# Attention on one core: TensorE's order in a unit grouped by the shape of the weights, masks as four 64x64 products, turned weights signalled by bank

## The reference

```python
B, H, S, D = 4, 8, 576, 64            # factor = 4, scale = 1 / sqrt(D)
q_d, k_d, v_d = (mean over 4 tokens of q, k, v)
out_up = np.repeat(sm_attn(q_d, k_d, v_d), factor, axis=2)
mask = np.abs(pos[:, None] - pos[None, :]) < factor
scores = np.where(mask, scale * np.matmul(q, k.transpose(0, 1, 3, 2)), -1000000000.0)
out_local = np.matmul(softmax(scores), v)
x = (out_up + out_local) as (B * S, H * D)          # 2304 x 512
x = (sigmoid(x @ w_gate) * (x @ w_val)) @ w_out     # d_ff 1536
h = x @ w_in; out = (h * sigmoid(1.702 * h)) @ w_out2   # d_ff 2048
```

## Time and profile before

| what | value |
|---|---|
| median of 3 runs | 871.63 us (871.37 to 872.4) |
| profiled execution | 872.51 us, span 870.8 us |
| TensorE busy | 857.5 us (98%) |
| VectorE, ScalarE, GpSimd busy | 624.1, 487.0, 589.2 us |
| six transposes of `turn` and of `turn_out`, mean ns of one | 282, 281 |
| granted TensorE clock, mean | 0.998 |

### The profile page before, as it was taken

How to read it: one execution, slowest core, us unless ns; L and a number is a source line. 1 busy time by engine, 2 the same in 40 slices (tenths; PEclk the granted TensorE clock), 3 DMA queues, 4 the chain that set the end, 5 groups by cost and what they waited for, 6 DMA issues and landing times.

```text
span 870.8 us, 18384 instructions
## 1 busy us (share of the span) xinstructions
PE 857.5 (98%) x6638; PEld 832.2 (96%) x6638; DVE 624.1 (72%) x1140; ACT 487.0 (56%) x1083; POOL 589.2 (68%) x471
## 2 busy tenths in 40 slices
PE   8989999999999999999999999999999999999998
PEld 6878899999999999999999999999999999999998
DVE  5767645555658685967676877777888778878777
ACT  5778754545536364645354646654676466556652
POOL 6688788888758648785457776763668644846523
PEclk9999999999999999999999999999999999999999
DMA  9877466685955787838588825345246751636432
GB/s 329 264 211 218 166 242 237 223 342 204 382 172 192 294 287 292 301 109 285 210 274 305 285 91 205 97 147 195 67 174 218 266 183 59 218 123 230 171 120 73
DMA packets 77369, 184.26 MB, mean 212 GB/s; under 512 B 5856, under 2 KB 31456, under 8 KB 74464
## 3 DMA queue, kind: packets, MB, share of 16 engines
q1 hardware_dynamic: 77280, 183.10, 60.2%
HBM read 141.66 MB, written 41.42 MB: 210 GB/s over the span
## 4 chain that ended last, share of the span: by engine, by line
PE 94%; issue 2%; DVE 1%; ACT 1%; POOL 1%; DMA 1%; SPq 0%; ACTq 0%; DVEq 0%
PE o_ps L808 10%; PE o_ps L809 10%; PE o_ps L810 10%; PE d_ps L662 7%; PE d_ps L664 7%; PE d_ps L663 7%; PE s_ps L662 6%; PE o_ps L653 6%; PE s_ps L664 6%; PE s_ps L663 6%; PE t_ps L662 3%; PE t_ps L663 3%; PE t_ps L664 3%; PE o_ps L626 2%; PE t_ps L597 1%
## 5 line engine op out<-in xcount | busy, mean ns | idle before, releaser
L808 PE MATMUL o_ps<-g_hi,v 128*128 128x384 f32 x504 | 169.6, 337 | 0.6 <-DVE att L1773 0.5
L809 PE MATMUL o_ps<-g_lo,v 128*128 128x384 f32 x504 | 169.4, 336 | 0.0
L810 PE MATMUL o_ps<-g_hi,v 128*128 128x384 f32 x504 | 169.4, 336 | 0.0
L1773 DVE TENSOR_TENSOR att<-o_ps,att 128x384 f32<-128x384 f32 x212 | 118.1, 557 | 56.4 <-PE o_ps L810 53.8
L2123 POOL TENSOR_TENSOR v<-v_f,v 128x512 fp32r<-128x512 f32 x72 | 95.0, 1340 | 56.2 <-ACT v L1076 56.2
L2123 POOL TENSOR_TENSOR v<-raw,v 128x512 fp32r<-128x512 f32 x54 | 70.9, 1312 | 89.8 <-ACT v L1069 77.2
L662 PE MATMUL d_ps<-xs_hi,w 128*128 128x384 f32 x360 | 121.0, 336 | 2.0 <-issue 1.2
L664 PE MATMUL d_ps<-xs_hi,w 128*128 128x384 f32 x360 | 120.5, 335 | 0.0
L663 PE MATMUL d_ps<-xs_lo,w 128*128 128x384 f32 x360 | 120.4, 335 | 0.0
L662 PE MATMUL s_ps<-xs_hi,w 128*128 128x384 f32 x300 | 101.2, 337 | 1.3 <-POOL xs_lo L2153 1.3
L664 PE MATMUL s_ps<-xs_hi,w 128*128 128x384 f32 x300 | 100.5, 335 | 0.0
(11 more groups left out here) (186 smaller groups left out, 2099.6 us busy)
## 6 DMA issues: line engine op xcount, KB each, us to landing
w<-w_split SPq DMA_DIRECT2D x48, 768.0 KB, 7.0
w<-w_split SPq DMA_DIRECT2D x48, 512.0 KB, 7.8
w<-w_split SPq DMA_DIRECT2D x96, 256.0 KB, 5.3
w_split<-w SPq DMA_DIRECT2D x12, 1792.0 KB, 6.7
raw<-in_w_out_dram SPq DMA_DIRECT2D x36, 512.0 KB, 4.5
w_split<-job_w SPq DMA_DIRECT2D x8, 1792.0 KB, 7.7
vw<-in_v_win_dram SPq DMA_DIRECT2D x16, 390.0 KB, 4.6
raw<-in_w_gate_val_dram SPq DMA_DIRECT2D x24, 256.0 KB, 3.3
```

Source lines behind the costliest of these rows:

```text
L808: pe.matmul(bank, vh, gh, start=(start and k == c), stop=False, skip_group_check=True)
L809: pe.matmul(bank, vh, gl, start=False, stop=False, skip_group_check=True)
L810: mm = pe.matmul(bank, vl, gh, start=False, stop=(k == c + 1), skip_group_check=True)
L1773: vec.tensor_tensor(part, value, part, ALU.add).then_inc(y_added, 1)
```

## The change

`masks(u)` makes four products for a unit, for each head one to each half of the output partitions (weights 64x64), in place of two with 64x128. In the loop, `score(i + 2)` goes ahead of `turn(i + 1)`, so that TensorE's order is weigh, masks, score, turn, turn_out. `turn` fills bank 1 first (pairs 4 and 5) and then bank 0, and signals after each; `copy_turned` copies in the same order, waits for each bank by itself and signals each copy. The values of `turned` and `copied` are doubled in the waits, and `weigh_pooled`, which writes only bank 1, waits for the copy of bank 1 alone.

```diff
@@ -327,7 +327,7 @@
                     sp.wait_ge(halved, u - QK_SLOTS + 1)
                     sp.wait_ge(scored, u - QK_SLOTS + 1)
                 if u > QK_SLOTS:
-                    sp.wait_ge(turned, u - QK_SLOTS)
+                    sp.wait_ge(turned, 2 * (u - QK_SLOTS))
                 sp.dma_start(qk[slot][:, 0, PAD:PAD + S], q_t[u]).then_inc(qk_loaded[slot], 16)
 
             def load_k(u):
@@ -535,9 +535,11 @@
             def masks(u):
                 if u >= 1:
                     pe.wait_ge(shifted, u)
-                for h in range(2):
-                    rows = slice(h * HK, (h + 1) * HK)
-                    pe.matmul(s_ps[:, h, 0:PAIRS * KW], picks[rows, :], mask[rows, :, :], start=True, stop=False)
+                for par in range(2):
+                    out_rows = slice(par * HK, (par + 1) * HK)
+                    for h in range(2):
+                        rows = slice(h * HK, (h + 1) * HK)
+                        pe.matmul(s_ps[out_rows, h, 0:PAIRS * KW], picks[rows, out_rows], mask[rows, :, :], start=True, stop=False)
 
             def score(u):
 
@@ -593,13 +595,14 @@
                     pe.wait_ge(copied_d, u)
                 if u >= 2:
                     pe.wait_ge(od_ready, u - 1)
-                for pair in range(PAIRS):
+                for pair in (*range(PT0, PAIRS), *range(PT0)):
                     mm = pe.transpose(t_ps[:, pair // PT0, (pair % PT0) * P:(pair % PT0 + 1) * P], e[:, pair, :, :].rearrange("p h k -> p (h k)"), ident[:, :])
-                mm.then_inc(turned, 1)
+                    if pair in (PT0 - 1, PAIRS - 1):
+                        mm.then_inc(turned, 1)
 
             def turn_pooled(u):
                 pe.wait_ge(normed_d, u + 1)
-                pe.wait_ge(copied, u + 1)
+                pe.wait_ge(copied, 2 * u + 2)
                 if u == 0:
                     pe.wait_ge(v_summed, 2)
                 if u >= 1:
@@ -631,7 +634,7 @@
                 pe.wait_ge(copied_d, u + 1)
                 pe.wait_ge(v_summed, u + 1)
                 if u + 1 < UNITS:
-                    pe.wait_ge(copied, u + 2)
+                    pe.wait_ge(copied, 2 * u + 3)
                 for c in range(2):
                     for h in range(2):
                         rows = slice(h * D, (h + 1) * D)
@@ -876,8 +879,8 @@
             for i in range(1, UNITS - 2):
                 weigh(i)
                 masks(i + 2)
+                score(i + 2)
                 turn(i + 1)
-                score(i + 2)
                 turn_out(i)
                 weigh_pooled(i)
                 sum_values(i + 2)
@@ -975,15 +978,14 @@
                                ).then_inc(v_summed, 1)
 
             def copy_turned(u):
-                act.wait_ge(turned, u + 1)
                 if u == 0:
                     act.wait_ge(sums_turned, 1)
                 if u >= 1:
                     act.wait_ge(weighed, u)
-                for b, pairs in enumerate((range(PT0), range(PT0, PAIRS))):
-                    c = nc.scalar.copy(p_t[:, 2 * pairs.start:2 * pairs.stop, 0:QW],
-                                       t_ps[:, b, 0:len(pairs) * P].rearrange("p (w k) -> p w k", k=HK)[:, :, 0:QW])
-                c.then_inc(copied, 1)
+                for n, (b, pairs) in enumerate(((1, range(PT0, PAIRS)), (0, range(PT0)))):
+                    act.wait_ge(turned, 2 * u + n + 1)
+                    nc.scalar.copy(p_t[:, 2 * pairs.start:2 * pairs.stop, 0:QW],
+                                   t_ps[:, b, 0:len(pairs) * P].rearrange("p (w k) -> p w k", k=HK)[:, :, 0:QW]).then_inc(copied, 1)
 
             def copy_turned_pooled(u):
                 act.wait_ge(turned_d, u + 1)
@@ -1539,7 +1541,7 @@
                 scores = s_ps[:, :, 0:PAIRS * KW].rearrange("p h (a k) -> p h a k", k=KW)
                 dve.wait_ge(maxed, u + 1)
                 if u >= 1:
-                    dve.wait_ge(turned, u)
+                    dve.wait_ge(turned, 2 * u)
                 vec.tensor_tensor(e[:, :, :, 0:KW].rearrange("p a h k -> p h a k"), scores,
                                   nmax[:, :].rearrange("p (h a) -> p h a", h=2).unsqueeze(3).broadcast_to([P, 2, PAIRS, KW]),
                                   ALU.add).then_inc(shifted, 1)
```

## The result

The changed kernel takes 872.72 us (median of 22 runs, 871.49 to 875.62), beside 871.57 us for the kernel before in as many runs taken with them; the ratio is 1.0020, with an interval of 1.0012 to 1.0029. So it is about 0.2% slower, where 867.0 was forecast and 864.8 to 869.7 was the range. Its profiled execution took 872.78 us, with a span of 870.0 us.

What follows compares the result with a forecast made beforehand. The prediction took TensorE, busy 857.5 of 870.8 us, as the bound. 13 units x 0.37 = 4.8 us, plus 0.3 outside the loop, less 0.5 for GpSimd, took 4.6 from 871.63 to 867.0 us; range 864.8 to 869.7.

Steps and rivals of the forecast that it cites:

- The drains: TensorE's unit: three of four changes of weight shape saved, 0.10 to 0.15 us each, 0.30 to 0.45 us a unit.
- Masks as four products: Masks group: four products run side by side in four array quarters, at no added time.
- rival (c): Masks group: the four products do not run side by side, 5 us slower, 876.8 us; chance 0.07.
- rival (b): Masks' borders: fp32 to bf16 weights cost like a shape change, so only one is saved, 869.6 us; chance 0.09.
- The unit of 5.67: Attention loop: an undisturbed unit falls from 6.04 to 5.67 us, 0.37 us less.
- a floor of T+2.27: turn_out waits for VectorE's normalise, earliest 2.27 us after weigh's start (T); a unit gains 0.38 us at most.
- Rival (d): Loop: normalise's chain, or ScalarE in units with castings, holds a unit near 5.9 us, 869.5 us; chance 0.09.
- The loads of the masks: Mask weights of 64 columns lose the fast load, estimated 53 ns each; 0.7 us if exposed, expected to be hidden.
- The clock: TensorE's clock was read as granted in full in every slice.
- GpSimd: Two units' turn_pooled wait for GpSimd's late pooled multiplication, 0.10 and 0.38 us; 0.5 us lost in all.
- rival (a): The 2.3 us instruction-fetch stall vanishes, 865.1 us, chance 0.14; or another joins, 869.3 us, chance 0.06.
- the sum: Whole kernel: 4.8 us from the loop, plus 0.3 outside, less 0.5 for GpSimd: 4.6 us gained.

Runs made afterwards that it cites:

- changed kernel without streams: The changed kernel with q and k loaded for four units only and both forms of v for two: 867.38 us, ratio 0.9960.
- masks alone: The kernel before with the four 64x64 mask products and without the new order: 870.25 us, ratio 0.9993.
- order alone: The changed kernel with the masks as two products again, keeping the new order, split copies and signals: 875.73 us, ratio 1.0049.
- orders before and after without streams: The kernel before and the changed kernel, q and k loaded for four units only, v's forms for two: 867.89 and 867.38 us.
- long pause: The changed kernel without streams, with the masks in the loop waiting for the end of VectorE's normalisation: 886.21 us, ratio 1.0169.
- 64 added products: The changed kernel with 64 small products (128 instructions) put once behind the first score, ahead of the loop: 875.39 us, ratio 1.0050.
- added loads: The kernel before with v's windows of units 3 to 15 loaded a second time into unused space: 874.48 us, ratio 1.0034.
- without v's windows: The changed kernel with v's windows loaded for the first two units only: 873.93 us, ratio 1.0034.

## Why the prediction was wrong

**Right, and in size.** The drains: 0.09 to 0.11 us less for weigh, masks and turn, 0.04 and 0.03 for score and turn_out. Masks as four products: 0.14 us for the group, so they run side by side, and rival (c), the slower side of the forecast, was wrong. bf16 weights ahead of fp32 ones of one shape cost nothing (0.14 us from masks to score), so rival (b) was wrong as well. The Trainium skill, "TensorEngine Tiling (Array Packing)", section "Key Properties", says that the array drains at a change of tiling mode and not between tiles of one mode; the trace agrees, across the two types too, with 0.75 us from weigh to masks where it was 0.86. The unit of 5.67; turn_out at T+2.30, beside a floor of T+2.27 that no wait shows at work. Rival (d) was wrong.

**The loads of the masks.** One load of 64x64 in bf16 has 107 ns in the records, one of 64x128 had 93. The Trainium skill, "TensorE: Matmul & The Clock Gate", section "Weight-path perf modes", gives the fast load only to weights of a full 128 columns. By the same page's section "LDWEIGHTS (loading the stationary operand)", P/1.2, an estimate for 64 columns is 53 ns; neither recorded time is as short. What counts is the row of PEld in the undisturbed unit, where all four start at 60.28, beside weigh's last products, and none delays the masks:

```profile
60.28 0.13 PEld L542 LDWEIGHTS s_ps<-mask,picks 64*64 64x64 bf16 x4
```

**The clock.** The prediction read it as granted in full in every slice. The mean of that execution is 0.998, and 0.72 from 5 to 10 us; a slice is too coarse to show it. No term of the sum hangs on this.

**GpSimd, a term that did not come.** 0.5 us was counted for it. The changed kernel shows no wait for it, probably because each gap gives it the rest that it lacked; in the changed kernel without streams, which has no gap near that unit, turn_pooled waits for it once, 0.3 us.

**The step that failed** is rival (a), and with it the sum, in which the stalls for instructions stand at no change. Rival (a) named the cause rightly, a stall for instructions whose place depends on where TensorE stands, and then priced it as one throw of a die: the one stall goes, 2.3 us gained, or one joins, 2.3 us lost, with 0.06 for the second. Two things were not seen. First, I had one wait of the trace, and did not ask how near all the other borders were to stalling. At five more borders of the kernel before, from 36 to 98 us, TensorE came to the border 2.35 to 2.8 us after the fetch had begun, where it needs some 2.4: these pieces came just in time (one of them 0.23 us late). Second, the change itself takes away what these borders had to spare: it makes the order quicker to execute and by that quicker to run out of program, and its fetches start later as well. The added instructions, on which I put it, bring no gaps by themselves (masks alone: 1.9 us in the loop, before 2.8), while the order alone has 5.0; together they have 8.3. The loop lost 5.5 us there, where rival (a) had 2.3, and that is more than the 4.8 us that its units gained.

**What is open.** Why a fetch starts when it does. In the orders before and after without streams it starts from 0.3 us ahead of the border to 3.3 us behind it, mostly with 30 to 150 instructions of the piece done; with streams up to 5.9 us behind (in order alone). Why it starts later in the new order with no data on the queues is not known, and this is the larger part of the difference there. That transfers delay it is shown only by leaving all streams out (mean 2.10 to 1.15 us before, 2.53 to 1.78 after); leaving out 390 KB a unit, or adding as much, moved the mean of the kernel before by only 0.1 us (to 1.99 and 2.17). Which transfers, and where they meet, no run shows. Orders that save the changes of shape and still spread the small products were not tried. None of the kernels that compute everything was faster than before by more than its interval.

## What to carry to other kernels

- On a TensorE that is busy throughout, read its stream a second way, by instructions per us. A wait for "issue" that returns at a fixed count of instructions is the program arriving late. Here a piece of 256 needed about 2.4 us from the start of its fetch, and the fetch mostly started 1 to 4 us into the piece before. Without data, the orders in which some 256 pass in 4.2 us or less stalled, and the one with 4.4 did not.
- Grouping equal shapes saves about 0.1 us for each drain, but many small products in a row spend the program fastest. Before joining two such groups, count the instructions in both. Keeping a group of few, long products between them may help where the kernel already shows such a wait; no run here tried it beyond the order before itself.
- A single wait in a trace is the visible end of a distribution. Ask for all places of its kind how much they have to spare before pricing it as chance.

## What was not expected of the hardware

After some pauses and some gaps the clock fell. In the kernel with the long pause TensorE stood 1.35 us ahead of the masks at 51.27, and from then on the same groups took, from start to start, 1.09 for score, 1.34 for turn and 1.32 for turn_out, where they took 0.78, 0.71 and 0.75 in the unit at 44.01:

```profile
51.27 0.34 PE L546 MATMUL s_ps<-mask,picks 64*64 64x336 bf16 x4 [1.35 <-DVE o_tok L1561]
51.44 1.17 PE L557 MATMUL s_ps<-qk 64*48 64x56 f32 x48
52.53 1.54 PE L603 MATMUL t_ps<-ident,e 128*128 128x128 f32 x6
53.87 1.39 PE L653 MATMUL o_ps<-ident,o_tok 128*128 128x128 f32 x6
55.19 0.71 PE L645 MATMUL t_ps<-pd_t,v_sum 128*64 128x144 f32 x8
```

The window of it, with the granted clock as the last column but two:

```profile
51.30:54.90 3.60, 3.60 (x63) 3.47 (x64) 1.66 (x3) 1.23 (x6) 1.65 (x4) 0.54 0.70 219
```

0.54 is the lower level, 1.2 GHz, for nearly all of these 3.6 us, and the three groups took 1.5 us more. Three units of this kernel have it; the unit at 44.01, with a pause as long, has not. The kernel with 64 added products has such a stretch behind three of its gaps (3.2, 1.4 and 2.0 us), order alone, the kernel with added loads and the changed kernel without v's windows behind one each. So a gap can cost more than its own length.

The changed kernel's profiled execution has no such stretch, not even behind its gap of 2.9 us. But of its 22 timed runs, 18 have a mean granted clock of 0.996 to 0.999 and four one of 1.00, while of the 62 runs of the kernel before that stand beside the experiments 57 have 1.00. The four have a median of 872.54 us, the fifteen with 0.998 one of 872.55, and the two with 0.996 took 874.1 and 875.5. So the clock does not make the result, and costs something only in single runs; where in these runs it fell was not recorded.

A load of 64x64 in bf16 is recorded no shorter than one of 64x128 (107 and 93 ns). Four products of 336 columns in four quarters take 0.14 us from the start of the first to that of the next group.
